# A fused attention, top-2 expert layer and tanh-gated MLP on one core: the expert stage in 20 tiles of 256 rows and 15 of 128 in place of 31 of 256

## The chip, the core and the metric

One core of a Trainium2 chip runs the whole program in one launch. The metric is the device time of the launch in microseconds; the median of three runs of the kernel before is 1261.28 us (1258.55 to 1262.38).

## What is computed

Three stages follow one another; all data is float32, and the result is 3072 x 384.

```python
# 1. linear attention with decay, B, H, S, D = 4, 8, 768, 48 -> x of 3072 x 384
state = w_t * state + outer(k_t, v_t);  y_t = r_t @ (previous state + outer(u * k_t, v_t))
# 2. experts: N, D, E, F = 3072, 384, 8, 1024
noisy = x @ w_gate + log1p(exp(x @ w_noise)) * noise
top2, weights = the two largest of the 8, softmax over them
out[token] += weight * (relu(x[token] @ w1[e]) @ w2[e])      # for each of its two experts
# 3. n_tokens, d_model, d_ff = 3072, 384, 2048
h = x @ w_in;  out = (h - tanh(h)) @ w_out
```

## The kernel before, in words

**Precision.** The products of the expert stage and of the last one are made of three products in a 32-bit format (fp32r) that TensorE takes in one pass: each operand is split into a high part (a copy into that format) and a low part (the operand less its high part), and hi x hi, hi x lo and lo x hi are added in the accumulation memory. ScalarE makes the high parts (`cp`, line 804; `h_hi` with the ReLU, line 947), VectorE the low parts (`sub`, line 1390; `h_lo`, line 1468). A weight matrix is thus loaded raw, then split in four pieces a tile: two halves of w1 (384 x 1024) and two of w2 (1024 x 384), each 128 x 1536 values.

**Routing.** Each token is written into the row buffer `xg` once for each of its two experts; an expert has a region of its own there (line 43, `REG`). The rows of an expert are cut into tiles. How many tiles each expert has is known only on the chip, so VectorE works out a table (`tables`, line 1173) that says for each tile its expert and its first row; a number of tiles that suffices for any distribution is run. Unused rows of the last tile of an expert are padding, for which `clear_pads` (line 409) writes zeros. The first NA = 5 tiles are chosen from the tokens of the first two batches, while the attention and the routing of the rest are under way (`early_1`, `early_2`); the others follow from `late_1` and `late_2` (lines 1236 and 1248). `shifts`, `shifted` and `slots_final` (lines 1251 to 1278) work out where each token's two result rows lie in `yg`.

**A tile.** There are NT = 31 tiles of T = 256 rows. On TensorE (`up`, `turn_tile`, `down`): 72 first products with 128 x 128 stationary weights and 256 moving columns into four banks of PSUM (2 to 5; bank b holds two of the eight blocks of the 1024 hidden values, 18 products each), then six transposes of the next tile's rows into banks 0 and 2, then 48 second products with the hidden values stationary and 384 columns of w2 moving, into banks 6 and 7. On ScalarE (`tile_act`, line 938), in this order: the high parts of w2 (two pieces), the high parts of the four banks of hidden values, the high parts of the next tile's w1 (two pieces) and of its rows, staging copies of the last stage's weights, the copy `y_out` of the results (line 961) and its store (line 963). VectorE (`tile_dve`, line 1461) follows with the low parts in the same order. SP (`tile_loads`, line 415) loads the next tile's rows, w1 and w2, each as soon as the single raw buffer of it has been read. There is one buffer of every kind: raw, high and low weights, rows and hidden values. The order on each engine is that in which the instructions are written; engines wait for one another through semaphores.

**What surrounds it.** In tiles 0 to 4 the routing of the last batch and the tables are put between the steps of the tiles by hand: a dictionary `between` names, for a tile and a place in it, what is to be done there; places 1 to 4 stand behind the four banks, 5 behind w1, 6 behind the rows. Sixteen of the later tiles also bring in 1/16 of the last stage's weights each (`st`). After the last tile, POOL gathers the two result rows of each token (line 1642), and the last stage begins.

Of the kernel before, what the change touches and what calls it, by code (L numbers as in the profile page):

```python
# [13 lines left out]
P = 128  # L14
# [4 lines left out]
DM = H * D  # L19
# [22 lines left out]
NT = (2 * N + E * (T - 1)) // T  # L42
REG = N + T
PAD_ROW = E * REG
ROWS = PAD_ROW + T
# [17 lines left out]
S0 = NA + 2  # L63


def build(nc, r, k, v, w, u, w_gate, w_noise, noise, w1, w2, w_in, w_out, out):
    ctx = ExitStack()
    with ctx:  # L68
        xg = nc.dram_tensor("xg", (ROWS, DM), F32, kind="Internal").ap()
        yg = nc.dram_tensor("yg", (NT * T, DM), F32, kind="Internal").ap()  # L70
# [27 lines left out]
        tile_tab = place("tile_tab", [1, 2, 32], I32)  # L98
        tick = place("tick", [P, 8])
        zero = place("zero", [P, 2, DM])  # L100
# [10 lines left out]
        step_b = place("step_b", [C, E])  # L111
        eoff = place("eoff", [C, E])
# [11 lines left out]
        xT_hi = place("xT_hi", [P, KD, T], F32R)  # L124
        xT_lo = place("xT_lo", [P, KD, T], F32R)
# [28 lines left out]
        tt = place("tt", [C, 4, 32 * E])  # L154
# [34 lines left out]
        tile_no = place("tile_no", [C, 32, E])  # L189
        tile_f = place("tile_f", [C, 32])  # L190
# [16 lines left out]
        stage_out = place("stage_out", [P, DM])  # L207
        offset[0] = region_m
# [44 lines left out]
        w1_raw_in = sem("w1_loaded"); w2_raw_in = sem("w2_loaded"); xt_loaded = sem("xt_loaded")  # L253
        w1_hi_s = sem("w1_hi_ready"); w1_lo_s = sem("w1_lo_ready"); w2_hi_s = sem("w2_hi_ready"); w2_lo_s = sem("w2_lo_ready")
        xT_full = sem("xT_full"); xT_hi_s = sem("xT_hi_ready"); xT_lo_s = sem("xT_lo_ready")
        h_full = sem("h_full"); h_hi_s = sem("h_hi_ready"); h_lo_s = sem("h_lo_ready")
        y_full = sem("y_full"); y_copied = sem("y_copied"); y_stored = sem("y_stored")
# [58 lines left out]
        def _(sp):  # L316
# [69 lines left out]
            for p in range(NP):  # L386
                next_w(p + 5)
                next_k(p + 4)
                next_v(p + 2)
                next_r(p + 4)  # L390
                if p == 4:
                    sp.wait_ge(tidied, TIDIED)
                    sp.dma_start(xg[PAD_ROW:PAD_ROW + T, :].rearrange("(a p) d -> p a d", p=P), zero[:]).then_inc(padded, 16)


            def load_w1(i):
                e = sp.value_load(tile_tab[0:1, 0, bass.ds(i, 1)], min_val=0, max_val=E - 1)
                sp.dma_start(w1_raw[:], w1[bass.ds(e, 1)].rearrange("o (c p) f -> p (o c) f", p=P)).then_inc(w1_raw_in, 16)

            def load_w2(i):  # L400
                e = sp.value_load(tile_tab[0:1, 0, bass.ds(i, 1)], min_val=0, max_val=E - 1)
                sp.dma_start(w2_raw[:], w2[bass.ds(e, 1)].rearrange("o (g p) d -> p (o g) d", p=P)).then_inc(w2_raw_in, 16)

            def load_x(i):
                row = sp.value_load(tile_tab[0:1, 1, bass.ds(i, 1)], min_val=0, max_val=PAD_ROW)
                sp.dma_start(xt_in[:], xg[bass.ds(row, T), :].rearrange("(a p) d -> p a d", p=P)).then_inc(xt_loaded, 16)


            def clear_pads():
                sp.wait_ge(counts_ready, 1)  # L410
                for e in range(E):
                    c0 = sp.value_load(cnt_i[0:1, e:e + 1], min_val=0, max_val=N)
                    sp.dma_start(xg[bass.ds(c0 + e * REG, T), :].rearrange("(a p) d -> p a d", p=P), zero[:]).then_inc(padded, 16)

            def tile_loads(i, st):

                if isinstance(i, int) and i == NA - 1:
                    sp.wait_ge(table_ready, 4)
                    sp.wait_ge(padded, 16 * (E + 1))
                    sp.wait_ge(scattered[1], 16 * JB * 2 * 2)  # L420
                reg_wait(sp, xT_full, i + 1)
                load_x(i + 1)
                reg_wait(sp, w1_lo_s, 2 * i + 2)
                load_w1(i + 1)
                if st is not None:
                    after(sp, stage_lo, 2 * st)
                    sp.dma_start(stage_in[:], w_in[:, bass.ds(st * P, P)].rearrange("(c p) f -> p c f", p=P)).then_inc(stage_in_s, 16)
# [12 lines left out]
            for i in range(NA - 1):  # L440
                tile_loads(i, None)
# [1228 lines left out]
```

## Time and profile before

| | |
|---|---|
| median of 3 runs | 1261.28 us |
| profiled execution, its own time | 1248.69 us |
| span of its trace, first to last instruction | 1247.0 us |
| mean granted TensorE clock, share of full speed | 0.945 |
| TensorE busy | 1174.9 us (94%) |
| VectorE busy | 717.1 us (58%) |
| ScalarE busy | 537.4 us (43%) |
| tile stage: first and last `y_out` copy | 265.0 and 808.3 us |
| moved by DMA | 179.87 MB, mean 144 GB/s |

The profile shows one execution. A line of a group names the source line, the engine (PE is TensorE, DVE VectorE, ACT ScalarE, SP the queue that starts loads), the operation, what it writes and reads with the shapes, and how often; then busy time, the mean of one and the idle time before. A TensorE product's duration contains its run through the array, and products overlap; how far their starts lie apart is what they cost. The granted clock is 1.00 at 2.4 GHz and 0.50 at 1.2 GHz.

### The profile page before, as it was taken

To read this page: it belongs to the slowest core of one execution; us is meant where nothing else is said; L and a number is where in the kernel's file an instruction comes from. 1 tells how busy PE (TensorE), PEld (TensorE's weight loads), DVE (VectorE), ACT (ScalarE), POOL (GpSimd) and SP (SyncE) were. 2 spreads that over 40 slices of the span, in tenths; PEclk is the share of its full clock that TensorE was granted. 3 is DMA by queue.
4 is the path that set the end of the run, shared out by engine and by line. 5 is a ranking of instruction groups with operands and counts; after the bars stand their busy time and mean duration, and the time that the engine had idled before them with its cause. 6 is when DMAs were issued, how large, how long until landed. Compare 5 with 4: busy or idle time off the path is not lost. (4 is left out here: it accounts for less than half of the span.)

```text
span 1247.0 us, 25009 instructions
## 1 busy us (share of the span) xinstructions
PE 1174.9 (94%) x9553; PEld 1142.7 (92%) x9553; DVE 717.1 (58%) x1047; ACT 537.4 (43%) x782; POOL 112.5 (9%) x140
## 2 busy tenths in 40 slices
PE   6898978897999999999999999949999999999998
PEld 5787867797999999999999999949999999999998
DVE  7979888748765756576666655523333333343433
ACT  5444533355355555556555555412322322223322
POOL 1000224213100000000000000030101101101010
PEclk8879778699999999999999999969999999999999
DMA  8445445365867777777676656520101101011010
GB/s 166 98 102 106 108 113 171 132 239 196 312 239 245 235 243 249 256 229 255 233 272 218 226 202 241 180 85 1 57 5 53 57 0 57 16 41 57 0 57 19
DMA packets 176523, 179.87 MB, mean 144 GB/s; under 512 B 96816, under 2 KB 159280, under 8 KB 176464
## 3 DMA queue, kind: packets, MB, share of 16 engines
q1 hardware_dynamic: 159152, 146.25, 37.5%
q0 software_dynamic: 6528, 20.06, 4.7%
q10 hardware_dynamic: 10784, 12.78, 2.8%
q8 instruction: 37, 0.61, 0.2%
q14 instruction: 22, 0.18, 0.0%
HBM read 149.18 MB, written 29.88 MB: 144 GB/s over the span
## 5 line engine op out<-in xcount | busy, mean ns | idle before, releaser
L1390 DVE TENSOR_TENSOR w_lo<-w_raw,w_hi 128x1536 fp32r<-128x1536 f32 x126 | 215.9, 1755 | 174.6 <-ACT w_hi L804 174.5
L686 PE MATMUL ps<-xT_hi,w_hi 128*128 128x256 f32 x744 | 213.6, 287 | 8.6 <-DVE xT_lo L1390 4.5
L687 PE MATMUL ps<-xT_lo,w_hi 128*128 128x256 f32 x744 | 212.6, 286 | 0.0
L688 PE MATMUL ps<-xT_hi,w_lo 128*128 128x256 f32 x744 | 212.5, 286 | 0.0
L1390 DVE TENSOR_TENSOR gg<-ps,th 128x768 f32<-128x768 f32 x64 | 61.3, 957 | 234.1 <-ACT th L1003 234.1
L804 ACT ACTIVATE w_hi<-w_raw 128x1536 fp32r<-128x1536 f32 x126 | 180.1, 1478 | 31.9 <-issue 25.0
L704 PE MATMUL ps<-w_hi,h_hi 128*128 128x384 f32 x496 | 168.9, 341 | 1.4 <-DVE h_lo L1468 1.4
L706 PE MATMUL ps<-w_hi,h_lo 128*128 128x384 f32 x496 | 166.2, 335 | 0.0
L705 PE MATMUL ps<-w_lo,h_hi 128*128 128x384 f32 x496 | 165.9, 334 | 0.0
L1003 ACT ACTIVATE th<-ps 128x768 f32<-128x768 f32 x64 | 52.0, 813 | 240.0 <-PE ps L755 240.0
L686 PEld LDWEIGHTS ps<-xT_hi,w_hi 128*128 128x128 f32 x744 | 144.7, 195 | 10.1 <-issue 7.8
L688 PEld LDWEIGHTS ps<-xT_hi,w_lo 128*128 128x128 f32 x744 | 144.8, 195 | 0.0
L687 PEld LDWEIGHTS ps<-xT_lo,w_hi 128*128 128x128 f32 x744 | 144.8, 195 | 0.0
L771 PE MATMUL ps<-wout_hi,g_hi 128*128 128x384 f32 x384 | 131.6, 343 | 0.0
L753 PE MATMUL ps<-x2T_hi,win_hi 128*128 128x384 f32 x384 | 130.3, 339 | 1.2 <-DVE x2T_lo L1390 1.2
L754 PE MATMUL ps<-x2T_lo,win_hi 128*128 128x384 f32 x384 | 130.2, 339 | 0.0
L755 PE MATMUL ps<-x2T_hi,win_lo 128*128 128x384 f32 x384 | 130.2, 339 | 0.0
L772 PE MATMUL ps<-wout_lo,g_hi 128*128 128x384 f32 x384 | 129.6, 338 | 0.0
L773 PE MATMUL ps<-wout_hi,g_lo 128*128 128x384 f32 x384 | 129.6, 337 | 0.0
L1642 POOL DMA_INDIRECT yy<-yg,slot_g x54 | 51.1, 946 | 828.3 <-DVE wt_g L1510 814.6
L947 ACT ACTIVATE h_hi<-ps 128x512 fp32r<-128x512 f32 x124 | 70.5, 591 | 87.1 <-PE ps L688 87.1
L1468 DVE SCALAR_TENSOR_TENSOR h_lo<-ps,h_hi 128x512 fp32r<-128x512 f32 x124 | 80.5, 685 | 29.7 <-ACT h_hi L947 29.4
(213 smaller groups left out, 1907.8 us busy)
## 6 DMA issues: line engine op xcount, KB each, us to landing
w_raw<-in_moe_w SPq DMA_DIRECT2D x64, 1536.0 KB, 6.6
xt_in<-xg SPq DMA_DIRECT2D x32, 384.0 KB, 5.1
yg<-y_out ACTq DMA_DIRECT2D x31, 384.0 KB, 4.8
k_pad<-in_k SPq DMA_DIRECT2D x32, 144.0 KB, 3.3
v_nat<-in_v SPq DMA_DIRECT2D x32, 144.0 KB, 3.3
out<-o_out SPq DMA_DIRECT2D x8, 576.0 KB, 4.0
w_nat<-in_w SPq DMA_DIRECT2D x15, 288.0 KB, 3.0
r_pad<-in_r SPq DMA_DIRECT2D x30, 144.0 KB, 2.8
```

The costliest lines, as they stand in the source:

```text
L686: pe.matmul(o, w1_hi[:, c, cols], xT_hi[:, c, :], start=first, stop=False, skip_group_check=True)
L687: pe.matmul(o, w1_hi[:, c, cols], xT_lo[:, c, :], start=False, stop=False, skip_group_check=True)
L688: mm = pe.matmul(o, w1_lo[:, c, cols], xT_hi[:, c, :], start=False, stop=(c == KD - 1), skip_group_check=True)
L704: pe.matmul(o, h_hi[:, f, cols], w2_hi[:, f, :], start=(f == 0), stop=False, skip_group_check=True)
L705: pe.matmul(o, h_hi[:, f, cols], w2_lo[:, f, :], start=False, stop=False, skip_group_check=True)
L706: mm = pe.matmul(o, h_lo[:, f, cols], w2_hi[:, f, :], start=False, stop=(f == FC - 1), skip_group_check=True)
L753: pe.matmul(o, win_hi[:, c, cols], x2T_hi[:, c, :], start=(c == 0), stop=False)
L754: pe.matmul(o, win_hi[:, c, cols], x2T_lo[:, c, :], start=False, stop=False)
L755: mm = pe.matmul(o, win_lo[:, c, cols], x2T_hi[:, c, :], start=False, stop=(c == KD - 1))
L771: pe.matmul(o, g_hi[p % 4][:, f2, cols], wout_hi[:, f, :], start=(f == 0), stop=False)
L804: nc.scalar.activation(dst, src, ACT.Copy).then_inc(s, 1)
L1390: vec.tensor_tensor(dst, a, b, ALU.subtract).then_inc(s, 1)
```

## The change

There are now NPAIR = 20 tiles of 256 rows and NSING = 15 of 128. Each expert's rows are cut into whole tiles, and what is left over goes to half tiles, as do whole tiles that would come after the twentieth. Tiles 0 to 4 are whole as before; behind them whole and half tiles take turns, 15 pairs of one of each, a whole one first.

- In a half tile, each first product has 256 moving columns: the high part of the 128 rows and their low part side by side (`xT_both`). With the high weights and with the low weights that makes 48 products in place of 72; it also adds lo x lo. The two halves of a bank are then two parts of the same sum: ScalarE copies the second to `h_part`, VectorE adds it to the first (`h_sum`), ScalarE makes the ReLU and high part out of `h_sum`, and VectorE the low part. There are 24 second products, three transposes, and `y_out` of half the size.
- w1 and w2 are loaded in halves with a semaphore for each half, about one tile further ahead. The split of w2 moves: its first half is split behind the next tile's w1, at the end of the tile before; its second half in the tile itself, behind bank 1.
- The tables get a third and a fourth part for the half tiles (`late_3`, `late_4`), `shifts` and `shifted` a third step, and their places move. Pads are cleared with 128 rows in place of 256.

The core of the diff; of the functions shown in full, the lines removed are those printed above.

```diff
-NT = (2 * N + E * (T - 1)) // T
-REG = N + T
+TS = T // 2
+NPAIR = (2 * N // TS - E) // 2
+NSING = (2 * N + E * (TS - 1)) // TS - 2 * NPAIR
+NT = NPAIR + NSING
+REG = N + TS
 PAD_ROW = E * REG
-ROWS = PAD_ROW + T
+ROWS = PAD_ROW + TS
+YS = NPAIR * T
...
+            def tile_loads(t, second, third, st):
+                if second is not None:
+                    reg_wait(sp, w2_lo_s, 2 * t.n + 2)
+                    load_w2(second, 1)
+                if third is not None:
+                    reg_wait(sp, xT_full, t.n + 2)
+                    load_x(third)
+                    for hf in range(2):
+                        reg_wait(sp, w1_lo_s, 2 * t.n + 3 + hf)
+                        load_w1(third, hf)
                 if st is not None:
+                    stage(st)
+                if third is not None:
+                    reg_wait(sp, w2_lo_s, 2 * t.n + 3)
+                    load_w2(third, 0)
...
+                            if t.one:
+                                both = ps[:, 2 + b, f2 * T:(f2 + 1) * T]
+                                pe.matmul(both, w1_hi[:, c, cols], xT_both[:, :, c, 0:TS], start=first, stop=False, skip_group_check=True)
+                                mm = pe.matmul(both, w1_lo[:, c, cols], xT_both[:, :, c, 0:TS], start=False, stop=(c == KD - 1),
+                                               skip_group_check=True)
+                                continue
...
+                    if f == FC // 2 - 1:
+                        mm.then_inc(y_half, 1)
...
+            with pe.Fori(0, NSING - 1) as i:
+                up(two_parts(i))
+                turn_tile(one_part(i))
+                down(two_parts(i))
+                up(one_part(i))
+                turn_tile(two_parts(i + 1))
+                down(one_part(i))
...
+            def w1_high(t, hf):
+                reg_wait(act, w1_raw_in[hf], 16 * t.n + 16)
+                follow(act, h_full, (FC // 2) * t.n - (2 if hf == 0 else 0))
+                cols = slice(hf * F // 2, (hf + 1) * F // 2)
+                cp(w1_hi[:, :, cols], w1_raw[:, :, cols], w1_hi_s)
+            def w2_high(t, hf):
+                reg_wait(act, w2_raw_in[hf], 16 * t.n + 16)
+                after(act, (y_half, y_full)[hf], t.n)
+                rows = slice(hf * FC // 2, (hf + 1) * FC // 2)
+                cp(w2_hi[:, rows, :], w2_raw[:, rows, :], w2_hi_s)
...
+            def second_part(t, b):
+                if b >= FC // 2:
+                    return
+                reg_wait(act, h_full, (FC // 2) * t.n + b + 1)
+                cp(h_part[b % 2][:], ps[:, 2 + b, :].rearrange("p (c k t) -> p c k t", c=2, k=2)[:, :, 1, :], h_parted)
+            def tile_act(t, nxt, st, step=lambda k_: None):
+                after(act, y_full, t.n)
                 step(0)
+                if t.one:
+                    second_part(t, 0)
                 for b in range(FC // 2):
+                    if t.one:
+                        second_part(t, b + 1)
+                        reg_wait(act, h_added, (FC // 2) * (t.at - NPAIR) + b + 1)
+                        nc.scalar.activation(h_hi[:, 2 * b:2 * b + 2, 0:TS], h_sum[b % 2][:], ACT.Relu).then_inc(h_hi_s, 1)
+                    else:
+                        reg_wait(act, h_full, (FC // 2) * t.n + b + 1)
+                        nc.scalar.activation(h_hi[:, 2 * b:2 * b + 2, :].rearrange("p c t -> p (c t)"), ps[:, 2 + b, :],
+                                             ACT.Relu).then_inc(h_hi_s, 1)
                     step(1 + b)
+                    if b == 1:
+                        w2_high(t, 1)
+                if nxt is not None:
+                    w1_high(nxt, 0)
+                    step(5)
+                    xT_high(nxt)
+                    w1_high(nxt, 1)
+                    step(6)
+                    w2_high(nxt, 0)
...
+                reg_wait(act, y_full, t.n + 1)
+                after(act, y_stored, 16 * t.n)
+                if t.one:
+                    nc.scalar.activation(y_out[:, 0, :], ps[:, 6, 0:DM], ACT.Copy).then_inc(y_copied, 1)
+                    reg_wait(act, y_copied, t.n + 1)
...
+                taken(whole_e, first_b, tiles_e, NPAIR)
+                seq(vec.tensor_tensor(whole_e[:], whole_e[:], used[:], ALU.add))
+                seq(vec.tensor_scalar(whole_e[:], whole_e[:], 2.0, None, ALU.mult))
+            def late_3():
+                over(tiles_e, N // TS, TS, 0)
+                seq(vec.tensor_tensor(tiles_e[:], tiles_e[:], whole_e[:], ALU.subtract))
+                run_on(first_c, tiles_e, NPAIR)
+                covered(first_c, NPAIR, NSING)
+                experts(NPAIR, NSING)
+            def late_4():
+                rows_of(first_c, NPAIR, NSING, TS, whole_e)
             def shifts():
...
+                for bound, step in ((bound_b, step_b), (bound_c, step_c)):
+                    seq(vec.tensor_scalar(slot_t[:], slot_f[:], bound[:, e:e + 1], step[:, e:e + 1], ALU.is_ge, ALU.mult))
+                    seq(vec.tensor_tensor(slot_y[:], slot_y[:], slot_t[:], ALU.add))
...
+            def both_parts(t, b):
+                if b >= FC // 2:
+                    return
+                v_.wait_ge(h_parted, (FC // 2) * (t.at - NPAIR) + b + 1)
+                v_.wait_ge(h_lo_s, (FC // 2) * t.n + max(b - 1, 0))
+                vec.tensor_tensor(h_sum[b % 2][:], ps[:, 2 + b, :].rearrange("p (c k t) -> p c k t", c=2, k=2)[:, :, 0, :],
+                                  h_part[b % 2][:], ALU.add).then_inc(h_added, 1)
+            def tile_dve(t, nxt, st, step=lambda k_: None):
+                if t.one:
+                    both_parts(t, 0)
                 for b in range(FC // 2):
+                    if t.one:
+                        both_parts(t, b + 1)
+                    v_.wait_ge(h_hi_s, (FC // 2) * t.n + b + 1)
+                    h_b = h_sum[b % 2][:] if t.one else ps[:, 2 + b, :].rearrange("p (c t) -> p c t", c=2)
+                    w = TS if t.one else T
+                    vec.scalar_tensor_tensor(out=h_lo[:, 2 * b:2 * b + 2, 0:w], in0=h_b, scalar=0.0, in1=h_hi[:, 2 * b:2 * b + 2, 0:w],
                                              op0=ALU.max, op1=ALU.subtract).then_inc(h_lo_s, 1)
                     step(1 + b)
+                    if b == 1:
+                        w2_low(t, 1)
+                if nxt is not None:
+                    w1_low(nxt, 0)
+                    step(5)
+                    xT_low(nxt)
+                    w1_low(nxt, 1)
+                    step(6)
+                    w2_low(nxt, 0)
...
-                       (2, 1): [lambda: placed(3), counts], (2, 2): [lambda: weights(3)], (2, 3): [late_1], (2, 4): [late_2],
-                       (3, 1): [shifts], (3, 3): [lambda: shifted(0), lambda: shifted(1)], (3, 4): [lambda: shifted(2), lambda: shifted(3)],
+                       (2, 1): [lambda: placed(3), counts], (2, 2): [lambda: weights(3)], (2, 3): [late[0]], (2, 4): [late[1]],
+                       (2, 6): [late[2]], (3, 1): [late[3]], (3, 3): [shifts], (3, 4): [lambda: shifted(0), lambda: shifted(1)],
+                       (3, 6): [lambda: shifted(2), lambda: shifted(3)],
```

## Rows read from the trace of the kernel before

**Rows 1.** Busy time by stretch, columns: us, PE, PEld, DVE, ACT, POOL, clock, DMA share, GB/s.

```profile
368.00:808.00 440.00, 440.00 (x3146) 439.82 (x3144) 271.83 (x282) 246.46 (x307) 0.00 (x0) 1.00 0.69 236
```

**Rows 2.** Waits from 350 to 800 us: who waited for whom, us in total, times, longest.

```profile
DVE w_lo L1390 <- ACT w_hi L804: 156.9, 51, 6.2
ACT y_out L961 <- PE ps L706: 110.5, 25, 5.0
```

**Rows 3.** Timeline of TensorE, one tile: start, duration, instruction.

```profile
702.22 0.28 PE L686 MATMUL ps<-xT_hi,w_hi 128*128 128x256 f32 x1
...
710.84 0.27 PE L665 MATMUL ps<-ident,xt_in 128*128 128x128 f32 x1
...
711.41 0.42 PE L704 MATMUL ps<-w_hi,h_hi 128*128 128x384 f32 x1
...
719.84 0.28 PE L686 MATMUL ps<-xT_hi,w_hi 128*128 128x256 f32 x1
```

**Rows 4.** Timeline of ScalarE: y_out copies, and one tile's splits.

```profile
367.62 0.81 ACT L961 ACTIVATE y_out<-ps 128x768 f32<-128x768 f32 x1 [4.95 <-PE ps L706]
...
702.53 0.81 ACT L961 ACTIVATE y_out<-ps 128x768 f32<-128x768 f32 x1 [4.95 <-PE ps L706]
...
711.10 0.60 ACT L947 ACTIVATE h_hi<-ps 128x512 fp32r<-128x512 f32 x1 [1.56 <-PE ps L688]
...
711.59 2.86 ACT L804 ACTIVATE w_hi<-w_raw 128x1536 fp32r<-128x1536 f32 x2
...
808.29 0.81 ACT L961 ACTIVATE y_out<-ps 128x768 f32<-128x768 f32 x1 [4.95 <-PE ps L706]
```

**Rows 5.** Groups by line and shape from 400 to 800 us: count, busy us, mean ns, idle before.

```profile
L1390 DVE TENSOR_TENSOR w_lo<-w_raw,w_hi 128x1536 fp32r<-128x1536 f32 x90 | 154.2, 1755 | 140.2 <-ACT w_hi L804 140.2
L804 ACT ACTIVATE w_hi<-w_raw 128x1536 fp32r<-128x1536 f32 x91 | 130.1, 1478 | 24.7 <-issue 23.9 <-ACT y_out L961 0.8
L1468 DVE SCALAR_TENSOR_TENSOR h_lo<-ps,h_hi 128x512 fp32r<-128x512 f32 x92 | 59.1, 684 | 13.3 <-ACT h_hi L947 13.3
L947 ACT ACTIVATE h_hi<-ps 128x512 fp32r<-128x512 f32 x92 | 51.9, 590 | 52.0 <-PE ps L688 52.0
L1390 DVE TENSOR_TENSOR xT_lo<-ps,xT_hi 128x256 fp32r<-128x256 f32 x23 | 9.6, 416 | 0.0
L804 ACT ACTIVATE xT_hi<-ps 128x256 fp32r<-128x256 f32 x22 | 8.5, 384 | 0.0
```

**Rows 6.** Timeline of VectorE, ahead of tile 3 and in one later tile.

```profile
309.69 1.00 DVE L1390 TENSOR_TENSOR xT_lo<-ps,xT_hi 128x512 fp32r<-128x512 f32 x2
...
711.73 0.69 DVE L1468 SCALAR_TENSOR_TENSOR h_lo<-ps,h_hi 128x512 fp32r<-128x512 f32 x1 [0.51 <-ACT h_hi L947]
...
713.11 3.43 DVE L1390 TENSOR_TENSOR w_lo<-w_raw,w_hi 128x1536 fp32r<-128x1536 f32 x2 [0.69 <-ACT w_hi L804]
...
716.45 1.02 DVE L1390 TENSOR_TENSOR xT_lo<-ps,xT_hi 128x512 fp32r<-128x512 f32 x2
```

**Rows 7.** Waits from 232 to 350 us.

```profile
PE ps L686 <- DVE xT_lo L1390: 4.5, 1, 4.5
```

**Rows 8.** Busy time by stretch around tiles 3 and 5, columns as in rows 1.

```profile
306.40:311.00 4.60, 0.20 (x1) 0.24 (x2) 4.60 (x6) 3.62 (x3) 3.99 (x3) 0.74 0.33 129
311.00:315.00 4.00, 4.00 (x20) 4.00 (x21) 3.03 (x2) 0.00 (x0) 3.86 (x1) 0.50 0.90 305
345.00:350.00 5.00, 3.89 (x23) 3.58 (x23) 4.28 (x5) 2.33 (x4) 0.00 (x0) 1.00 0.40 148
```

**Rows 9.** Groups of VectorE from 285 to 350 us.

```profile
L1390 DVE TENSOR_TENSOR w_lo<-w_raw,w_hi 128x1536 fp32r<-128x1536 f32 x12 | 20.5, 1749 | 6.3 <-ACT w_hi L804 6.3
L1468 DVE SCALAR_TENSOR_TENSOR h_lo<-ps,h_hi 128x512 fp32r<-128x512 f32 x12 | 8.1, 685 | 3.1 <-ACT h_hi L947 2.7 <-DVE slot_y L1270 0.2
L1270 DVE TENSOR_TENSOR slot_y<-slot_y,slot_t 128x48 f32<-128x48 f32 x8 | 1.7, 209 | 0.3
L1205 DVE TENSOR_TENSOR tt<-tt,used 128x216 f32<-128x216 f32 x1 | 0.4, 384 | 0.0
```

More of the change, by code:

```diff
@@ L1 @@
+from collections import namedtuple
 from contextlib import ExitStack
@@ L62, with whole, two_parts, one_part @@
 NA = -(-(2 * 2 * S - E * (T - 1)) // T)
-S0 = NA + 2
+assert NPAIR - NA == NSING and NT <= 39
+Tile = namedtuple("Tile", "one n at xs")
+def whole(k):
+    return Tile(False, k, k, 2 * k)
+def two_parts(i):
+    return Tile(False, NA + 2 * i, NA + i, 2 * NA + 3 * i)
+def one_part(i):
+    return Tile(True, NA + 2 * i + 1, NPAIR + i, 2 * NA + 3 * i + 2)
 def build(nc, r, k, v, w, u, w_gate, w_noise, noise, w1, w2, w_in, w_out, out):
@@ L123, in build @@
         xt_in = place("xt_in", [P, 2, DM])
-        xT_hi = place("xT_hi", [P, KD, T], F32R)
-        xT_lo = place("xT_lo", [P, KD, T], F32R)
+        xT_both = place("xT_both", [P, 2, KD, T], F32R)
+        xT_hi, xT_lo = xT_both[:, 0], xT_both[:, 1]
         h_hi = place("h_hi", [P, FC, T], F32R)
@@ L207, in build @@
         stage_out = place("stage_out", [P, DM])
+        h_part = two(place, "h_part", [P, 2, TS])
+        h_sum = two(place, "h_sum", [P, 2, TS])
         offset[0] = region_m
@@ L1211, in rows_of, with over, taken, run_on @@
                 vec.tensor_copy(tile_tab[0:1, 1, lo:lo + rows], tile_f[0:1, 0:rows]).then_inc(table_ready, 1)
+            def over(dst, M, size, offset):
+                seq(vec.tensor_scalar(r3(0, M), tile_no[:, 0:M, :], float(size), float(offset), ALU.mult, ALU.add))
+                seq(vec.tensor_tensor(r3(2, M), b8(total, M), r3(0, M), ALU.is_gt))
+                seq(vec.tensor_reduce(dst[:], r3(2, M).rearrange("o t e -> o e t"), AX.X, ALU.add))
+            def taken(dst, first, tiles, limit):
+                seq(vec.tensor_scalar(dst[:], first[:], -1.0, float(limit), ALU.mult, ALU.add))
+                seq(vec.tensor_scalar(dst[:], dst[:], 0.0, None, ALU.max))
+                seq(vec.tensor_tensor(dst[:], dst[:], tiles[:], ALU.min))
+            def run_on(first, tiles, begin):
+                seq(vec.tensor_tensor_scan(last_e[:], ones[:, 0:E], tiles[:], float(begin), ALU.mult, ALU.add))
+                seq(vec.tensor_tensor(first[:], last_e[:], tiles[:], ALU.subtract))
             def early_1():
```

366 lines of the change are left out of this document (179 added, 187 removed).

## Prediction

> **What bounds the kernel now.** I read the busy time by stretch first, then the waits of the expert stage, then one tile instruction by instruction on TensorE, ScalarE and VectorE. From 368 to 808 us TensorE is busy in every microsecond at full clock, while VectorE and ScalarE are busy for 272 and 246 of the 440 us and the DMA engines for 0.69 [rows 1]. All long waits of this stretch are those of ScalarE for TensorE and of VectorE for ScalarE; TensorE has none [rows 2]. So the 25 tiles between the y_out copies at 367.62 and 808.29 take 440.67/25 = 17.63 us each [rows 4], and this is TensorE time: 72 first products from 702.22 to 710.84 (8.62 us, 0.120 each), six transposes to 711.41 (0.57), 48 second products to 719.84 (8.43, 0.1735 each and about 0.1 at the start) [rows 3]. ScalarE and VectorE have a slack of 7 us in each tile. That slack is what the change spends.
>
> **The change, TensorE's part.** A half tile has 48 first products of 256 columns, 48 x 0.120 = 5.75 us, and 24 second products, 24 x 0.1735 + 0.1 = 4.25 us. The transposes are 0.28 us for a half tile and 0.57 for a whole one; each tile turns the next. A pair is then 8.62 + 0.28 + 8.43 + 5.75 + 0.57 + 4.25 = 27.90 us. Tiles 0 to 4 stay whole. Behind them stood 26 tiles, 26 x 17.62 = 458.1 us; now there are 15 pairs, 418.5 us. If TensorE never waited, the gain would be 39.6 us.
>
> **What a half tile asks of the other two.** The weights are split anew for each tile, whatever its rows. VectorE: four w_lo of 1.755 us, ScalarE: four w_hi of 1.478 [rows 5]. Back to back, two cost 3.43 and 2.86 [rows 4, 6]. The half tile adds for each of four banks a ScalarE copy and a VectorE add of 256 columns, and keeps a ReLU and an h_lo of 256. No row has these four; the nearest are the 256 wide xT_hi (0.384 us) and xT_lo (0.416) [rows 5], and I take 0.40 and 0.42. Bounds: 0.38 below; above, what the 512 wide h_hi and h_lo take, 0.59 and 0.68 [rows 5]. I take the low ones, since they have the same width. The 256 wide moving operand now comes from two blocks of 128; I cost it at the 0.120 us of an unbroken one, with 0.1735, the 384 wide pitch, as the far bound (48 x 0.054 = 2.6 us a tile); it has the width of the row at 0.120, so that is nearest.
>
> **The half tile in order.** Let 0 be the end of its first products on TensorE. ScalarE sees bank 2 at -1.18 us (the last bank takes 1.44, and the notice 0.26 with the run-out of the last product). Copy to -0.80, ReLU of bank 1 to -0.45. Now comes the second half of w2: w_hi to 0.97, and behind it on VectorE w_lo from 1.00 to 2.76. VectorE issues in order, so the add of bank 3 stands behind this w_lo: to 3.10. ReLU of bank 3 to 3.55, h_lo of bank 2 to 3.44 and of bank 3 to 4.00. Only then ScalarE starts w1 of the next tile: w_hi to 4.95, w_lo to 6.74, xT_lo pair (1.02 [rows 6]) to 7.70, and the next tile's first products may start at 7.75. TensorE meanwhile turns (0.57), makes half the second products by 2.74, waits for h_lo of bank 2 until 3.50, ends at 5.58, and waits until 7.75. So it idles 0.76 + 2.17 = 2.93 us in each pair. Rows of before show the hand-overs that I used: h_lo starts 0.03 us after h_hi ends (711.70, 711.73), y_out 0.1 to 0.2 after the last product [rows 4, 6].
>
> **The whole tile in order.** With 0 at its start: the rest of the previous work leaves VectorE at 3.3; banks come at 2.2, 4.3, 6.5 and 8.6; h_lo of bank 2 is done at 8.9 and of bank 3 at 10.2, against 13.1 and 15.2 when the second products reach them; w1's first half and xT_lo of the half tile are ready at 13.2, w1's second half at 14.8, w2's first half at 16.7, the staging copies at 17.7. TensorE reaches 17.33. No wait; the slack of 4 us here cannot be lent to the half tile, since w1_hi is written only after the h banks of the tile before.
>
> **Queues.** SP now waits in the order w2 second half, x, w1 halves, staging, w2 first half. Each wait is for a w_lo or a turn, and what is queued behind it is needed over 8 us later: w2's second half of the half tile is asked for at 8.3 us of the whole tile and used at 22.5, w1 of the next whole tile at 12.7 and used near 26. A pair moves about 6.3 MB of weights and 1.6 MB of rows, results and staging: 7.9 MB in 30.8 us, 256 GB/s against 236 now [rows 1]; from 311 to 315 us 305 were moved [rows 8]. I cost the loads at nothing. POOL's queue is not touched here.
>
> **Sum of the pairs.** 15 x (27.90 + 2.93) = 462.5 us; the last half tile has no next tile to wait for, -2.2: 460.3. Against 458.1: +2.2 us. Hand-overs I have left out (register waits, the loop's end) could be 0 to 0.3 us a pair; I take 0.1, +1.5. The last copy and store are half as big: the copy took 0.81 [rows 4], so -0.5.
>
> **Tiles 0 to 4.** VectorE makes the tables. About 49 small instructions come in (22 in the third and fourth part, 5 behind the second, 6 shifts, 16 steps) at 0.21 us for 48 columns and 0.38 for 216 [rows 9], some 12 us, less 1.5 for narrower tables. Against that, the order is better: up to now tile 3 could not start for 4.5 us, since both w_lo of w1 stood behind the tables and ahead of xT_lo [rows 7]; now its first half and xT_lo go ahead of the third part. Following VectorE down its list from 285 us, where it has 6.3 + 3.1 us to spare before w_lo and h_lo [rows 9], I get the start of tile 3 at 306.3 against 310.7 [rows 6], and of tile 5 at 349.6, against 349.8 (the y_out copy at 367.62 less a tile's 17.62 and the hand-over). Net 0, between -4 and +4.
>
> **The clock.** After tile 3's 4.5 us of waiting the granted clock was 0.74 and then 0.50 (1.2 instead of 2.4 GHz), and back at 1.00 later; with 1.1 us of TensorE idle between 345 and 350 it stayed 1.00 [rows 7, 8]. The 2.17 us foreseen lie between. The 4.0 us of work at 0.50 from 311 to 315 cost 2.0 us, and a little on each side of them: I price one fall at 2.3 us, and count it in one pair of four, since a gap half as long should halve the clock less often, 15 x 0.25 x 2.3 = +8.6. The bounds are none and all: 0 and 34.5. The Trainium skill (TensorE: Matmul & The Clock Gate, HAM oscillation — how this bites in real kernels) ties the halved clock to an idle gap longer than this one; by it this term would be 0. That the clock fell after 4.5 and not after 1.1 us agrees with it and doesn't decide.
>
> The whole: 2.2 + 1.5 - 0.5 + 0 + 8.6 = +11.8 us on the profiled execution's 1248.69, 1260.5. The median of the runs is 1261.28, 1.0% above that execution; by the same ratio 1260.5 becomes 1273, and with the uncertain clock term I say 1272.
>
> **Rivals.** (A) The forecast, 1262 to 1282: chance 0.45.
> (B) The waits as above, but the clock never falls: +3.2 us, 1264.5, and by the error of the 2.93 us (0.3 a pair) from 1259 to 1269. For it: the gap is half of the one that did it. 0.22, most of it within 0.3%.
> (C) The clock falls in every second pair or in all: +3.2 + 17 to 35 us, 1282 to 1300. For it: two gaps, 0.76 and 2.17, lie 2 us apart. [...] 0.15.
> (D) Faster: the place of the w2 split doesn't matter. If the chain of the half tile were only bank 3's copy, add, ReLU and h_lo (to 1.9), then w_hi, w_lo and xT_lo (to 6.0), the wait would be 1.2 us a pair: 15 x 29.1 - 1.2 - 458.1 = -23, 1239; with no wait at all -40, 1220. For it: in total VectorE has 22 us of work for 30 us of pair. Against it: the order of the instructions, which is fixed, and VectorE's w_lo waits of 157 us [rows 2], which show that it follows ScalarE. 0.18 with the case that tiles 0 to 4 gain over 4 us.
>
> **Numbers.** A measurement of this kernel tells 0.3% (3.8 us) from no change. Faster: D, 0.18. Same: most of B and the edge of A, 0.22. Slower: 0.60. The range of 8 in 10 leaves out D and the top of C: 1250 to 1292; A's own is 1262 to 1282.
>
> **What would show it.** Right: in the changed profile TensorE idle of about 2.2 us before the first product of each whole tile, released by VectorE's xT_lo, and 0.8 us ahead of the fifth pair of second products, released by h_lo; y_out copies 30.8 us apart for a pair; starts of pair 0 near 349. The clock term: granted clock under 1.00 in some stretches between 350 and 810. Wrong: pairs of 28 to 29 us (then D), a wait for w_raw (then loads), or a pitch of the half tiles' first products above 0.12.

## The result, and the profile after

| | changed kernel | kernel before, beside it |
|---|---|---|
| median | 1336.88 us (1336.34 to 1337.63, 4 runs) | 1261.83 us (1258.55 to 1262.59, 4 runs) |
| ratio, with its 95% interval | 1.060 (1.058 to 1.062) | |
| profiled execution, span | 1337.63 us, 1336.1 us | [table above] |
| mean granted clock | 0.931 | 0.945 |

The change makes the kernel 75 us slower. The direction was the forecast one; 1272 us and the range of 1250 to 1292 are far off.

The copies `y_out` first. Line 1061 is that of the whole tiles (tile 4 and the 15 pairs), line 1056 that of the half tiles; behind the three durations stand the first and the last start:

```profile
L1061 ACT ACTIVATE y_out<-ps x16: 789/792/812, 352.8 to 877.6; 128x768 f32<-128x768 f32 x16
L1056 ACT ACTIVATE y_out<-ps x15: 472/488/499, 397.1 to 889.0; 128x384 f32<-128x384 f32 x15
```

From tile 4's copy to the last one it takes 889.0 - 352.8 = 536.2 us, where the kernel before took 808.3 - 348.9 = 459.4. A pair takes (889.0 - 397.1)/14 = 35.1 us; 30.8 were forecast, and 31.4 with the clock's share. Tile 4's copy itself is only 4 us late, and so is that of tile 0 already (269.1 against 265.0); from one to the other it takes 83.8 us in both kernels.

The waits from 377 to 870 us answer to [rows 2]: who waited for whom, us in total, times, longest. TensorE had no row there; now it has the two large ones shown and one of 3.7 us, and the longest wait of all is a new one, ScalarE's for a load:

```profile
ACT win_hi L873 <- DMA stage_in<-in_moe_w_in: 102.5, 14, 8.2
DVE win_lo L1521 <- ACT win_hi L873: 90.5, 15, 7.1
ACT h_hi L1036 <- PE ps L748: 74.7, 53, 3.4
...
PE ps L721 <- DVE h_lo L1617: 43.2, 14, 4.1
...
PE ps L746 <- DVE xT_both L1521: 29.7, 14, 2.3
```

One pair shows how the three hang together. First the timeline of SP's queue: start, duration, instruction:

```profile
618.73 2.42 SPq L429 DMA_DIRECT2D w_raw<-in_moe_w  x2
621.48 0.37 SPq L452 DMA_DIRECT2D stage_in<-in_moe_w_in  x1
```

The same microseconds on ScalarE, with the idle time before an instruction and what ended it in brackets:

```profile
618.57 1.49 ACT L873 ACTIVATE w_hi<-w_raw 128x1536 fp32r<-128x1536 f32 x1 [0.76 <-PE ps L768]
627.55 0.53 ACT L873 ACTIVATE win_hi<-stage_in 128x384 f32 x1 [7.49 <-DMA stage_in<-in_moe_w_in]
628.07 0.53 ACT L873 ACTIVATE wout_hi<-stage_out 128x384 f32 x1
628.50 0.79 ACT L1061 ACTIVATE y_out<-ps 128x768 f32<-128x768 f32 x1
...
630.12 0.66 ACT L873 ACTIVATE h_part<-ps 128x256 f32<-128x256 f32 x2 [0.83 <-ACT y_out L1061]
```

And TensorE's instructions that had to wait, of the half tile that follows:

```profile
632.08 0.44 PE L721 MATMUL ps<-ident,xt_in 128*128 128x128 f32 x2 [3.26 <-DVE h_lo L1617]
636.12 0.41 PE L766 MATMUL ps<-w_hi,h_hi 128*128 128x384 f32 x1 [1.37 <-DVE h_lo L1617]
640.77 0.47 PE L746 MATMUL ps<-xT_both,w_hi 128*128 128x256 f32 x1 [2.30 <-DVE xT_both L1521]
```

ScalarE is ready for the staging copy at 620.06. The load is asked for at 621.48, behind both halves of w1 (1.57 MB), and the copy starts at 627.55, when it has landed. ScalarE takes its instructions in the order in which they are written, so `y_out` of the whole tile and the first `h_part` of the half tile stand behind it, although the whole tile's second products ended near 622.5. TensorE ends the half tile's first products near 628.3 and waits 3.26 us in the middle of turning the next tile, because no `h_lo` is there yet. The 2.30 us at the end are the forecast wait for xT_lo.

Busy time by stretch, columns as in [rows 1]:

```profile
622.50:628.30 5.80, 5.80 (x50) 5.80 (x49) 0.06 (x1) 0.75 (x2) 0.00 (x0) 1.00 0.93 323
628.30:632.10 3.80, 0.54 (x6) 0.30 (x4) 2.19 (x5) 2.60 (x8) 0.00 (x0) 1.00 0.32 114
...
640.80:645.00 4.20, 4.20 (x23) 4.20 (x23) 2.79 (x2) 0.82 (x3) 0.00 (x0) 0.59 0.75 250
645.00:650.00 5.00, 5.00 (x44) 5.00 (x43) 2.44 (x3) 2.95 (x4) 0.00 (x0) 1.00 0.86 300
380.00:870.00 490.00, 415.00 (x2720) 403.10 (x2721) 300.24 (x344) 265.13 (x371) 0.00 (x0) 0.93 0.66 217
```

The DMA engines are busy (323 GB/s) just while ScalarE waits, and do little in the next stretch. Behind the three waits the granted clock is 0.59, mostly its lower level; over the stage it is 0.93, where it was 1.00 [rows 1]. One such fall takes 0.41 x 4.2 = 1.7 us of full clock, the whole stretch lacks 0.07 x 490 = 34, as much as 20 falls in its 14 pairs. Some of that falls into microseconds in which TensorE waits anyway and costs nothing.

Why was this wait not there before? There SP asked for w1 of tile i+1, and behind it for the staging of tile i, when tile i was about to begin, and the copies stood near its end. SP's queue and ScalarE in one tile of the kernel before:

```profile
471.85 0.37 SPq L427 DMA_DIRECT2D stage_in<-in_moe_w_in  x1
```

and

```profile
485.94 0.54 ACT L804 ACTIVATE win_hi<-stage_in 128x384 f32 x1
```

That is 14 us of room for the load. The old `tile_loads` for tile i waited for the w1_lo of tile i, made at the end of tile i-1; the new one waits for that of the next tile, made at the end of the tile that runs. The staging argument is still that of tile i, so its load moved from the start of the tile to its end, and the copies stayed there.

### The profile page after: what moved, and what is told of

Same layout as the page of the kernel before. It is cut to its first block and busy times, and to the rows that moved or that the text cites. A ratio compares the mean times of both kernels' runs of the same rounds, so it can differ in the third digit from the quotient of the medians.

```text
span 1336.1 us, 25734 instructions
## 1 busy us (share of the span) xinstructions
PE 1170.5 (88%) x9286; PEld 1124.0 (84%) x9286; DVE 770.3 (58%) x1177; ACT 570.3 (43%) x867; POOL 108.8 (8%) x140
## 5 line engine op out<-in xcount | busy, mean ns | idle before, releaser
L1521 DVE TENSOR_TENSOR w_lo<-w_raw,w_hi 128x1536 fp32r<-128x1536 f32 x140 | 244.3, 1755 | 55.8 <-ACT w_hi L873 52.1
L873 ACT ACTIVATE w_hi<-w_raw 128x1536 fp32r<-128x1536 f32 x140 | 205.7, 1483 | 24.4 <-PE ps L768 16.8
L746 PE MATMUL ps<-xT_both,w_hi 128*128 128x256 f32 x480 | 144.1, 300 | 38.7 <-DVE xT_both L1521 36.9
L767 PE MATMUL ps<-w_lo,h_hi 128*128 128x384 f32 x440 | 155.7, 354 | 0.4 <-issue 0.4
L768 PE MATMUL ps<-w_hi,h_lo 128*128 128x384 f32 x440 | 155.2, 353 | 0.0
L748 PE MATMUL ps<-xT_both,w_lo 128*128 128x256 f32 x480 | 141.7, 295 | 0.0
L747 PE MATMUL ps<-xT_both,w_hi 128*128 128x256 f32 x480 | 141.6, 295 | 0.0
L746 PEld LDWEIGHTS ps<-xT_both,w_hi 128*128 128x128 f32 x480 | 98.3, 205 | 44.4 <-issue 42.2
L824 PE MATMUL ps<-x2T_hi,win_lo 128*128 128x384 f32 x384 | 130.1, 339 | 0.0
L766 PEld LDWEIGHTS ps<-w_hi,h_hi 128*128 128x128 f32 x440 | 89.9, 204 | 10.6 <-issue 7.9
L747 PEld LDWEIGHTS ps<-xT_both,w_hi 128*128 128x128 f32 x480 | 98.3, 205 | 0.0
L748 PEld LDWEIGHTS ps<-xT_both,w_lo 128*128 128x128 f32 x480 | 98.1, 204 | 0.0
L1036 ACT ACTIVATE h_hi<-ps 128x512 fp32r<-128x512 f32 x80 | 47.6, 597 | 114.4 <-PE ps L748 113.1
```

The source lines that it names most:

```text
L746: pe.matmul(o, w1_hi[:, c, cols], xT_hi[:, c, 0:w], start=first, stop=False, skip_group_check=True)
L747: pe.matmul(o, w1_hi[:, c, cols], xT_lo[:, c, 0:w], start=False, stop=False, skip_group_check=True)
L748: mm = pe.matmul(o, w1_lo[:, c, cols], xT_hi[:, c, 0:w], start=False, stop=(c == KD - 1), skip_group_check=True)
L766: pe.matmul(o, h_hi[:, f, cols], w2_hi[:, f, :], start=(f == 0), stop=False, skip_group_check=True)
L824: mm = pe.matmul(o, win_lo[:, c, cols], x2T_hi[:, c, :], start=False, stop=(c == KD - 1))
L873: nc.scalar.activation(dst, src, ACT.Copy).then_inc(s, 1)
```

## The experiments

Ratios are to runs of the kernel before on the same chip. A pair is the distance of the first and last half tile's `y_out`, over 14, each from that kernel's own row like the one above. The last of the 14 is 1 to 3 us shorter than most in the faster runs, because no tile follows its half tile, so the pairs between take a little more than the mean.

| run | median us | ratio (95%) | pair us |
|---|---|---|---|
| changed kernel | 1336.88 | 1.060 (1.058 to 1.062) | 35.1 |
| e1_stage_first | 1270.26 | 1.010 (1.006 to 1.014) | 31.3 |
| e2_thin_w2 | 1238.84 | 0.985 (0.981 to 0.989) | 29.1 |
| e3_nops | 1338.30 | 1.063 (1.060 to 1.067) | 35.4 |
| e4_narrow | 1256.66 | 0.998 (0.997 to 1.000) | 30.4 |
| e5_reorder | 1233.00 | 0.993 (0.989 to 0.996) | 29.8 |
| e7_nops_64 | 1232.67 | 0.991 (0.989 to 0.994) | 29.8 |
| e8_addresses | 1235.64 | 0.993 (0.990 to 0.996) | 29.8 |
| e9_w1_third | 1231.06 | 0.989 (0.984 to 0.995) | 29.7 |
| e10_reorder_only | 1319.16 | 1.060 (1.055 to 1.066) | 35.2 |
| e11_copies_later | 1278.53 | 1.017 (1.015 to 1.019) | 31.1 |
| c_before | 1242.96 | 1.000 (0.996 to 1.004) | |
| c_after | 1324.51 | 1.064 (1.053 to 1.075) | 35.6 |

**The staging loads first (e1_stage_first).**

```
             def tile_loads(t, second, third, st):
+                if st is not None:
+                    stage(st)
...
-                if st is not None:
-                    stage(st)
```

> The changed kernel, with the two staging loads asked for at the start of a tile's loads instead of behind the loads of w1. Theory S (staging: ScalarE sits 7.3 us of each pair behind the late stage_in, so y_out of the whole tile and all that follows in the half tile is late, which is most of TensorE's 3.3 us at the half tile's turn and feeds the falls of the clock): the wait of win_hi on the load is gone, the first wait of the half tile drops from 3.3 to about 0.8 us, a pair takes 31 to 32.5 us instead of 35.1, and the time is 1277 to 1300 us. Theory N (the half tile's own chain of copies, sums, ReLU and low parts is the limit and covers the staging): at most 10 us gained, 1327 or more. Theory C (TensorE's clock falls once per pair whatever the first wait is): the wait goes, but the granted clock of 380 to 890 us stays at 0.93 and the time above 1300.

68 us are back against e3_nops, which ran beside it. Theory S holds: ScalarE's wait for the load is gone and a pair takes 31.3 us. Two of its numbers were too cautious: the first wait was to drop to 0.8 us and is gone, and 1270 us lies below its 1277 to 1300. Its copies `y_out`:

```profile
L1061 ACT ACTIVATE y_out<-ps x16: 810/812/812, 349.1 to 809.6; 128x768 f32<-128x768 f32 x16
L1056 ACT ACTIVATE y_out<-ps x15: 487/489/492, 382.9 to 821.1; 128x384 f32<-128x384 f32 x15
```

TensorE's waits from 377 to 830 us:

```profile
PE ps L746 <- DVE xT_both L1521: 31.4, 14, 2.3
PE ps L766 <- DVE h_lo L1617: 9.3, 15, 1.2
```

Busy time by stretch: behind the half tile of one of the longer pairs, and over the pairs:

```profile
601.90:606.00 4.10, 4.04 (x23) 4.05 (x24) 3.05 (x3) 1.34 (x3) 0.00 (x0) 0.67 0.78 251
...
380.00:810.00 430.00, 391.60 (x2742) 383.77 (x2743) 300.39 (x343) 265.32 (x368) 0.00 (x0) 0.99 0.77 248
```

The wait at the turn is gone, not only smaller; what is left is 2.2 us for xT_lo and 0.6 for h_lo a pair. The clock still falls, but in one pair of four or five: eleven of the 14 pairs take 31.3 us or less and three 32.7, and 0.01 x 430 = 4.3 us of full clock are lacking, about three falls (the stretch shown has 0.33 x 4.1 = 1.4 us of one, which ends a little behind it).

Of the 3.8 us a pair that this edit gives, 2.6 are idle time of TensorE: 490 - 415.0 = 75.0 us in 14.0 pairs of the changed kernel, 430 - 391.6 = 38.4 us in 13.7 pairs here. The other 1.2 are busy time, 29.7 us a pair against 28.5 for the same instructions, and the only difference that the profile shows in them is the granted clock. Theory C falls: most falls went with the long first wait.

How long is such a load under way? From the issue to the landing of `stage_in`, in the kernel before, in the changed kernel and in e1_stage_first:

```profile
DMA to landing us min/median/max: 5.7/6.0/6.8
DMA to landing us min/median/max: 4.8/5.3/6.6
DMA to landing us min/median/max: 5.4/6.3/8.1
```

So the load is not slow in the changed kernel, not even behind 1.57 MB of w1; it is asked for too late. In e1_stage_first SP asks 11.7 us ahead of the copy:

```profile
606.67 0.37 SPq L452 DMA_DIRECT2D stage_in<-in_moe_w_in  x1
...
618.33 0.50 ACT L873 ACTIVATE win_hi<-stage_in 128x384 f32 x1
```

**The loads late, the copies later (e11_copies_later).** In the loop over the pairs and behind it, on both engines:

```
-                tile_act(two_parts(i), one_part(i), i + 1)
-                tile_act(one_part(i), two_parts(i + 1), None)
+                tile_act(two_parts(i), one_part(i), None)
+                tile_act(one_part(i), two_parts(i + 1), i + 1)
```

> The changed kernel with its loads in their old order; only ScalarE's two staging copies and VectorE's two subtractions are moved from the end of the whole tile to the end of the half tile behind it, some 12 us later. If the cost of the staging is that ScalarE, which works in order, stands behind a late load with y_out and the half tile's chain behind it, this is as good as e1_stage_first: no wait on stage_in, 31 to 32.5 us a pair, 0.76 to 0.82 hundredths of the change's 6 taken back, that is 1.01 to 1.02 times the kernel before. If it is the order of the loads themselves (staging behind w1 delays w1, w2 or x), the pair stays at 34 us or more and the ratio at 1.05 or more. Rival between them: the copies (1.0 us of ScalarE, 1.1 of VectorE) now stand in the tile in which both engines have least room, and cost 0.5 to 1 us a pair, 1.02 to 1.03.

SP's list is that of the changed kernel to the letter, and the ratio is 1.017. So the order of the loads costs nothing by itself; it costs because ScalarE stands behind one of them with urgent work. ScalarE waits for stage_in once from 377 to 830 us, in pair 0, whose copies were not moved:

```profile
ACT win_hi L873 <- DMA stage_in<-in_moe_w_in: 7.0, 1, 7.0
```

A pair takes 31.1 us. The ratio is 0.7 hundredths (9 us) above that of e1_stage_first: pair 0 ends 12.5 us later, at 395.4 instead of 382.9 (2.1 of it are there at tile 4's copy already), and the 14 behind it take together 3.5 us less. So the copies cost nothing in the half tile.

**The order of the half tile (e10_reorder_only, e5_reorder, e9_w1_third).** In `tile_act`, and alike in `tile_dve`; in e9 the first half of w1 stands at `b == 2`, everything else as here. e5 and e9 also have the staging loads first, as in e1_stage_first; e10 does not:

```
                 if t.one:
+                    w2_high(t, 1)
                     second_part(t, 0)
...
                     if b == 1:
-                        w2_high(t, 1)
+                        if not t.one:
+                            w2_high(t, 1)
+                        elif nxt is not None:
+                            w1_high(nxt, 0)
                 if nxt is not None:
-                    w1_high(nxt, 0)
+                    if not t.one:
+                        w1_high(nxt, 0)
```

> As e5_reorder but with the staging loads asked for where the change has them, behind the loads of w1. It tells whether the late staging load costs by itself what e1_stage_first gave back, or only together with a full chain behind it. If y_out of the whole tile is as late as in the changed kernel (ScalarE behind stage_in for 7 us), TensorE still waits at the half tile's turn, 2.5 to 4 us a pair, and the clock falls with it: 33 to 35 us a pair in pairs with staging, 1290 to 1325 us. If the shorter chain absorbs it: 30 to 31 us a pair, below 1255.

> As e1_stage_first, and in half tiles the split of the second half of w2 stands ahead of the first bank, and that of the next tile's first half of w1 right behind the second bank instead of behind the fourth, on ScalarE and VectorE alike; all the work is still done. e1_stage_first takes 31.2 us a pair, of which TensorE waits 2.2 for xT_lo and 0.6 for h_lo. If only the order of the chain makes these waits (both engines have less work in a half tile than TensorE, 10.4 us of VectorE beside 10.6), a pair takes 28.0 to 29.2 us and the time is 1222 to 1240 us, and no fall of the clock is left between 400 and 780 us. Rival: both engines are so full in a half tile that the wait only moves to the next tile (w_lo or h_lo there): a pair stays above 30 us and the time above 1250.

> As e5_reorder, with the split of the next tile's first half of w1 behind the third bank instead of the second. There TensorE waited 1.4 us a pair for h_lo of the third bank, because VectorE worked on w1_lo (1.76 us) ahead of its sum. If that is the whole of the rest, the wait drops below 0.5 us, a pair takes 28.7 to 29.3 us instead of 30.1, and the time is 12 to 21 us below e5_reorder (3 to 4 hundredths of the kernel before less 0.7). Rival: w1_lo or xT_lo are then late for the next tile's first products, 1 us or more per pair, and the time is within 6 us of e5_reorder.

Without timely staging the other order gives nothing (35.2 us a pair, 1.060): TensorE's waits only gather at the turn, 77 us in all, as much as the three of the changed kernel together (43.2 + 29.7 + 3.7). The first case of the expected text held, though the wait is nearly 6 us a pair where 2.5 to 4 were expected. With timely staging the other order gives 1.5 us a pair and 1.7 hundredths. TensorE's waits of e10_reorder_only, 385 to 860 us:

```profile
PE ps L721 <- DVE h_lo L1623: 76.9, 13, 8.0
```

Those of e5_reorder, 380 to 780 us:

```profile
PE ps L766 <- DVE h_lo L1623: 18.1, 13, 1.4
PE ps L721 <- DVE h_lo L1623: 3.1, 13, 0.2
```

Its busy time in that stretch:

```profile
380.00:780.00 400.00, 378.77 (x2667) 370.78 (x2667) 292.45 (x333) 257.05 (x358) 0.00 (x0) 1.00 0.81 259
```

The waits of e9_w1_third, 380 to 780 us:

```profile
PE ps L766 <- DVE h_lo L1623: 12.0, 13, 1.0
PE ps L721 <- DVE h_lo L1623: 3.1, 13, 0.3
```

e5_reorder's 1233 us lie in the expected 1222 to 1240, but by luck: that range lies 30 to 48 us below e1_stage_first's 1270, on a chip where the kernel before takes 1259 us, and on this chip it takes 1245. Its ratio of 0.993 makes 1250 us of 1259. Nor does the pair hold: the pairs between the first and the last take 30.1 us instead of 28.0 to 29.2. Both lie where the rival put them, at the edge of its 30 us and 1250. What did come true is that no wait for xT_lo is left and no fall of the clock; in their place w1_lo now delays h_lo of the third bank by 1.4 us. Moved one bank on (e9), it delays that of the fourth by 0.9, the pairs between take 29.9 us, and the gain is too small to tell; of e9's expected text the rival's number held and not its mechanism. Wherever a w_lo of 1.76 us stands in the half tile, something of 0.4 us that TensorE wants stands behind it. e5_reorder and e9_w1_third beat the kernel before beside them, by 0.7 and 1.1 hundredths, with intervals that end below 1. All the work is done in them.

**What the split of w2 costs in the chain (e2_thin_w2).**

```
 def w2_high(t, hf):
...
-                cp(w2_hi[:, rows, :], w2_raw[:, rows, :], w2_hi_s)
+                m = 16 if t.one and hf else DM
+                cp(w2_hi[:, rows, 0:m], w2_raw[:, rows, 0:m], w2_hi_s)
```

VectorE's subtraction gets the same bound.

> As e1_stage_first, and in half tiles ScalarE's copy and VectorE's subtraction of the second half of w2 touch only 16 of 384 columns (the rest of that half keeps older values; this part of the split is left out). This takes about 1.3 us of ScalarE and 1.6 us of VectorE out of the middle of the half tile's chain. Theory N and the prediction's own term (the chain behind up of a half tile makes TensorE wait 2.9 us a pair, partly for this split): 1.5 to 2.5 us per pair less than e1_stage_first, 22 to 38 us in all, more where the clock then stays up. If the chain is not what TensorE waits for: within 5 us of e1_stage_first.

2.2 us a pair less than e1_stage_first, 31 us in all, and the wait for xT_lo falls from 2.2 to 1.2 us (16.9 us in 14 times), that for h_lo to nothing. The split of w2 does stand in the chain that TensorE waits for, as the forecast had it.

**Narrow first products (e4_narrow).** The branch of `up` for half tiles, `second_part` and `both_parts` are taken out; ReLU and h_lo read the bank's first 256 columns.

> As e1_stage_first, and the half tiles' first products are 72 of 128 columns instead of 48 of 256, so that both parts of the rows need no second copy and no sum: ScalarE loses 4 copies of 0.37 us and VectorE 4 sums of 0.42 us per half tile, and the chain of a bank two hand-overs. What 128-column products take no row of the two traces shows; if 0.08 to 0.107 us, up takes 5.8 to 7.7 us instead of 5.75. Theory N (the chain is the limit): the chain's saving wins, 1 to 2 us per pair less than e1_stage_first (15 to 30 us). Theory W (TensorE's own work is the limit, which is what the wide form was made for): up to 2 us per pair more.

Three of its products of 128 columns, 0.333 us from one w_lo product to the next:

```profile
617.00 0.28 PE L740 MATMUL ps<-xT_both,w_hi 128*128 128x128 f32 x1
617.33 0.28 PE L740 MATMUL ps<-xT_both,w_hi 128*128 128x128 f32 x1
617.66 0.28 PE L740 MATMUL ps<-xT_both,w_hi 128*128 128x128 f32 x1
```

So 0.111 us for 128 columns beside 0.120 for 256, and 72 x 0.111 = 8.0 us instead of 5.75. TensorE then does not wait (378 of the 380 us from 400 to 780 are busy). It pays 2.3 us more for the first products and saves 2.8 of waiting and the falls of the clock: 0.9 us a pair, 13.6 us in all, a little less than theory N's 15.

**The last stage (e3_nops, e7_nops_64, e8_addresses, c_before, c_after).** The profile of the changed kernel has a last stage 9.4 us longer than that of the kernel before, in code that the change does not touch. The second tanh of a group starts 4.4 us behind the first instead of 3.1:

```profile
1018.67 0.81 ACT L1104 ACTIVATE th<-ps 128x768 f32<-128x768 f32 x1 [1.83 <-PE ps L824]
1023.05 0.81 ACT L1104 ACTIVATE th<-ps 128x768 f32<-128x768 f32 x1 [3.56 <-PE ps L824]
```

> The changed kernel with 24 empty instructions on ScalarE ahead of the last stage, nothing else. Theory P (the last stage is 9.4 us longer than before although its code is the same, because ScalarE's loop lies at another place in its instruction stream and one fetch in each pass comes late): the period of a group goes from 52.6 us to another value, at best the 51.3 us of before, and the second tanh of a group starts 3.1 instead of 4.4 us behind the first; the time moves by up to 9 us with the expert stage as it was. Theory D (what is long there comes from the data or the memory: other rows gathered, other places in the buffers): period and time as they were, within 2 us.

24 empty instructions ahead of ScalarE's part of the last stage move nothing: 52.5 us a group, 4.35 us between the two.

> As e5_reorder, with 64 empty instructions on ScalarE and 64 on TensorE ahead of the last stage. 24 on ScalarE left the group's period at 52.5 us (51.3 in the kernel before). If the place of either loop in its instruction stream makes it, a shift this large should move the period or the gap between the first two tanh of a group (4.4 us, 3.1 before). If not, both stay within 0.1 us.

> As e5_reorder, with the buffers of the last stage at the addresses that they had before the change (1312 bytes higher) and the added semaphores allocated behind all others, so that those of the last stage have their old numbers but one group. If addresses or semaphore numbers make the second tanh of each group 1.25 us late, the gap goes back to 3.1 us and the last stage gets 9 us shorter; if the place in the instruction stream does, it stays at 4.4.

Both, and e5_reorder too, which has neither edit, took 51.3 us a group (e8: 51.7) with 3.1 us between the two. So these two runs test nothing: they ran on a chip where the late tanh does not occur. That led to the pair of plain kernels on one chip.

> The kernel before, unedited, for a profile from the same chip as those beside it. Its median was 1259 us beside the first four experiments and 1245 us beside the next three, on another chip, and a group of the last stage took 52.5 us in the profiles of the former and 51.3 in those of the latter, whatever the edit. If the chip makes this difference and not the change, this run and the changed kernel beside it show the same period and the same gap between the first two tanh of a group, either 51.3 and 3.1 us or 52.5 and 4.4. If the change makes it, this run shows 51.3 and the changed kernel 52.5.

> The changed kernel, unedited, beside the kernel before on one chip. By the chip theory its last stage is as long as that of the kernel before in the run beside it, and all of the difference of some 76 us lies ahead of it, in the expert stage. By the other its last stage is 9 us longer.

The changed kernel on the other chip (c_after), for the rows above:

```profile
1021.59 0.81 ACT L1104 ACTIVATE th<-ps 128x768 f32<-128x768 f32 x1 [1.74 <-PE ps L824]
1024.71 0.81 ACT L1104 ACTIVATE th<-ps 128x768 f32<-128x768 f32 x1 [2.31 <-PE ps L824]
```

3.12 us, 51.3 a group, as in c_before beside it. The same changed kernel shows both values, so the difference goes with the chip and not with the change; the kernel before was never profiled on a chip with 4.4 us. The last stages of c_before and c_after are equally long, so what the change costs lies ahead of the last stage.

## Why the prediction failed, point by point

**The step that failed** is the part "Queues". It set down SP's order rightly, staging behind both halves of w1, and then said that what is queued behind each wait "is needed over 8 us later" and "I cost the loads at nothing". It gave examples for w1 and w2 and none for staging, which is asked for 1.4 us after ScalarE is ready for it and lands 6 us later. In "The whole tile in order" the staging copies were put at 17.7 us by VectorE's work alone, with no arrival of their data. The runs showed a wait of ScalarE of 7.3 us a pair (102.5/14) in its place. From tile 4's copy to the last, the stage takes 536.2 us with it and 821.1 - 349.1 = 472.0 in e1_stage_first without it, so the term that was put at nothing measured 64 us, with the falls of the clock that hang on it. e11_copies_later, with the loads as late and the copies later, takes 830.1 - 351.2 = 478.9: 10.4 us more than e1_stage_first in pair 0, where the wait is left, and 3.5 less behind it.

**The chain of the half tile** was right. With the staging in time the stage takes 472.0 us, and the forecast had 459.4 + 11.8 = 471.2. That these two are so near is in part luck: the clock took 4.5 us where 8.6 were forecast, and the pairs without a fall 0.3 us more each. Wait for xT_lo: 2.17 forecast, 2.24 measured. Wait for h_lo: 0.76 and 0.62. A pair without a fall of the clock: 30.93 with the 0.1 for hand-overs, and 31.23. The ratio that the prediction gave, 1272/1261.28 = 1.009, is that of e1_stage_first (1.006 to 1.014), of another kernel than the one to be forecast.

**The pitch** of the 256 wide product over two blocks: taken as 0.120 us and measured so. Copies and sums: 0.40 and 0.42 forecast, 0.38 and 0.42 measured.

**The clock.** One fall in four pairs at 2.3 us was the forecast. In e1_stage_first it is three in 14, at 32.7 - 31.23 = 1.5 us each; in the changed kernel, with 3.1 us of waiting ahead of the rest, as much as 20 in 14 pairs. With waits of at most 1.4 us (e5_reorder) it never fell. In the pair shown of e1_stage_first, behind a wait of 2.25 us with one of 0.56 some 4.6 us ahead of it, the clock was 0.67 for the next four; behind like waits in eleven other pairs it did not fall, and why it falls in some is open. The rule of the Trainium skill (TensorE: Matmul & The Clock Gate, HAM oscillation — how this bites in real kernels), by which this term would have been 0, disagrees with the trace.

**Tiles 0 to 4.** Net 0, between -4 and +4, was forecast. From tile 0's copy to tile 4's it takes 83.8 us in the changed kernel, 83.7 in e1_stage_first and 83.8 in the kernel before: net 0. The 4 us by which the changed kernel's copies come later are there at tile 0's.

**The rivals.** A gave the size of a kernel with timely staging. C came nearest in its mechanism, many falls, but ends at 1300. D, that the order of the splits might not matter, fell with e2_thin_w2 (2.2 us a pair) and e5_reorder (1.5). What none of them had was a load that is late for an engine off the critical path. The prediction named its sign, "a wait for w_raw (then loads)", for the weights alone.

**The scaling by 1%** from the profiled execution to the median: on two chips the kernel before has its median at 1259 and 1257 us with 52.5 us a group in the runs beside it, on two others at 1245 and 1243 with 51.3. Its profiled execution, 1248.69 us with 51.3, fits the latter and its other runs the former; that it came from such a chip is argued, not shown.

## What to carry to other kernels

When the loop over tiles is shifted against the loads, list for every load, the small ones too, when it is asked for, how long it takes to land (here 5 to 8 us, wherever it stood in the queue), and when the first engine in program order wants it; a load of 0.2 MB that feeds nothing urgent costs as much as one that does if the copy out of its buffer stands ahead of urgent work. An idle wait on an engine with slack is free only as long as nothing behind it in its list is on the path: move such copies behind the urgent ones, or ask for their data a tile earlier. And shorten the chain only once that wait is gone, since before it nothing is gained.

## What was not expected of the hardware

On two of four chips the second tanh of each group started 4.4 us behind the first, on the others 3.1, in the same code and at equal TensorE pitch (0.52 us from one of the L824 products to the next); a group takes 52.5 or 51.3 us, some 9 us of the kernel. The products that it reads had ended on time by the trace, and ScalarE had been idle for 3.5 us. 24 empty instructions ahead did not move it; the cause is open, and so is whether the chip itself makes it or something else that differed between these sessions.

With new 128 x 128 weights for each, a product of 128 columns takes 0.111 us against 0.120 for one of 256, so a half as wide moving operand saves 8%, not half.

In e8_addresses each step of the last stage took 6.35 us instead of 6.29, 3.3 us from the first tanh to the last (400.3 instead of 397.0). Its buffers lie 1312 bytes higher than in e5_reorder, but the kernel before has them at the same addresses and takes 6.29, so the addresses alone do not make it; the order of the semaphores was changed too. This was not followed up.
